# The operands of the first layers stand at four other distances from the weights in SBUF

## What is computed

```python
w = softmax(weight_gen)                     # per token: 8 heads, 7 taps
x = sum over 7 taps of w * x[token - tap]   # causal mixing, per head of 24 columns
y = ((sigmoid(x @ w_gate)) * (x @ w_val)) @ w_out       # 192 -> 1536 -> 192
h = y @ w_in                                            # 192 -> 2048
g = (a0 + a1*h + a2*h*h + a3*h*h*h) / (1 + |b0|*|h| + |b1|*h*h + 1e-6)
out = g @ w_out2                                        # 2048 -> 192
```

## Time and profile before

| | |
|---|---|
| median of 3 runs | 1399.78 us (1399.17 to 1400.05) |
| the profiled execution's own time | 1399.86 us |
| its span, first to last instruction | 1398.1 us |
| busy: TensorE, its weight loads, VectorE, ScalarE, GpSimd | 97%, 88%, 90%, 77%, 26% |

### The profile page before, as it was taken

The page is one execution under the profiler, slowest core; times in us unless marked ns, Lnnn a source line. Parts: engine busy times, 40 slices in busy tenths (PEclk is TensorE's granted clock), DMA queues, the critical chain, the costliest instruction groups (busy, mean ns, idle before and its releaser), DMA issues.

```text
span 1398.1 us, 19047 instructions
## 1 busy us (share of the span) xinstructions
PE 1362.1 (97%) x7282; PEld 1234.8 (88%) x7282; DVE 1257.5 (90%) x1498; ACT 1080.7 (77%) x1467; POOL 356.9 (26%) x204
## 2 busy tenths in 40 slices
PE   5999999999999999999999999999999999999977
PEld 5899899899899899999999998998998999999966
DVE  7788999999999999999999999999998998889998
ACT  3487887787888787787778878788777778778975
POOL 0333233141332323133141323323133231210000
PEclk9999999999999999999999999999999999999999
DMA  9200100001010010101001010010101001000000
GB/s 231 76 32 1 38 0 23 22 1 43 1 44 1 0 44 0 44 1 34 10 1 44 0 43 1 0 44 0 42 1 40 1 1 35 1 12 0 13 0 18
DMA packets 13467, 33.06 MB, mean 24 GB/s; under 512 B 1600, under 2 KB 7746, under 8 KB 13376
## 3 DMA queue, kind: packets, MB, share of 16 engines
q1 hardware_dynamic: 13312, 31.85, 7.5%
q0 software_dynamic: 64, 0.00, 0.0%
HBM read 25.55 MB, written 6.29 MB: 23 GB/s over the span
## 4 chain that ended last, share of the span: by engine, by line
PE 91%; DVE 5%; ACT 1%; issue 1%; DMA 0%; SPq 0%; DVEq 0%
PE ring L325 50%; PE acc L352 40%; PE ring L379 1%; PE ring L382 1%; DVE work L734 1%; DVE work L713 1%; DVE work L707 1%; DVE work L720 1%; DVE work L743 0%; DVE work L727 0%; DVE work L654 0%; DMA window<-in_x_dram 0%; DVE u L701 0%; ACT work L500 0%; DVE val_w L671 0%
## 5 line engine op out<-in xcount | busy, mean ns | idle before, releaser
L352 PE MATMUL acc<-out_w,work 128*128 128x192 f32 x2048 | 365.8, 330 | 13.8 <-DVE work L743 13.8
L352 PEld LDWEIGHTS acc<-out_w,work 128*128 128x128 f32 x2048 | 341.8, 192 | 20.1 <-DVE work L743 14.1
L490 ACT ACTIVATE work<-ring,coef 128x512 f32<-128x512 f32 (+1 forms) x272 | 182.2, 670 | 215.4 <-PE ring L325 212.9
L325 PE MATMUL ring<-yt,in_w 128*128 128x512 f32 (+1 forms) x1360 | 326.0, 386 | 2.3 <-DVE work L713 1.9
L352 PE MATMUL acc<-out_w,u 128*128 128x192 f32 x1536 | 283.8, 327 | 3.7 <-DVE u L701 3.5
L325 PEld LDWEIGHTS ring<-yt,in_w 128*128 128x128 f32 x1360 | 244.9, 189 | 47.5 <-DVE work L713 2.9
L352 PEld LDWEIGHTS acc<-out_w,u 128*128 128x128 f32 x1536 | 256.7, 190 | 9.7 <-DVE u L701 3.3
L325 PE MATMUL ring<-xt,gate_w 128*128 128x512 f32 (+1 forms) x1020 | 262.3, 387 | 1.3 <-DVE val_w L671 0.8
L325 PE MATMUL ring<-xt,val_w 128*128 128x512 f32 (+1 forms) x1020 | 252.2, 377 | 0.0
L604 POOL TENSOR_TENSOR mixed<-mixed,prod 128x768 f32<-128x768 f32 (+1 forms) x90 | 197.2, 2191 | 169.0 <-DVE u L701 152.1
L599 POOL TENSOR_TENSOR prod<-window,mixw 128x768 f32<-128x768 f32 (+1 forms) x90 | 135.3, 1503 | 399.3 <-DVE work L720 298.0
(11 more groups left out here) (57 smaller groups left out, 915.8 us busy)
## 6 DMA issues: line engine op xcount, KB each, us to landing
window<-in_x_dram SPq DMA_DIRECT2D x14, 960.0 KB, 4.7
out_dram<-zsb SPq DMA_DIRECT2D x15, 384.0 KB, 2.6
out_w<-in_moe_w_out_dram SPq DMA_DIRECT2D x1, 1536.0 KB, 21.2
mixw<-in_weight_gen_dram SPq DMA_DIRECT2D x13, 112.0 KB, 3.0
out_w<-in_moe_w_out_dram SPq DMA_DIRECT2D x2, 576.0 KB, 8.2
work<-in_moe_w_in_dram SPq DMA_DIRECT2D x2, 512.0 KB
work<-in_moe_w_in_dram SPq DMA_DIRECT2D x4, 256.0 KB, 14.5
window<-in_x_dram SPq DMA_DIRECT2D x1, 768.0 KB, 4.3
```

The costliest lines, as they stand in the source:

```text
L325: last = nc.tensor.matmul(dst, wt[:, c], xs[:, 0:n], start=at == 0, stop=at == 4)
L352: last = nc.tensor.matmul(dst, src[:, n * P:(n + 1) * P], w[:, i, :], start=i == 0 and n % 2 == 0, stop=i == last_i and n % 2 == 1, skip_g ...
L490: nc.scalar.activation(den(n), h, ACT.Abs, scale=coef[:, 6:7])
```

## The change

No instruction is added, removed or moved. The tensors `xt0_free`, `xt1_free`, `yt0_free`, `yt1_free` and `work_free` are never read or written; they push what stands behind them. 

```diff
-        xt = [[sb(f"xt{b}_{n}", [P, T], F32R) for n in range(4)] for b in range(2)]
-        yt = [[sb(f"yt{b}_{n}", [P, T], F32R) for n in range(4)] for b in range(2)]
+
+        def operands(name, free):
+            sb(f"{name}_free", [P, free // 4])
+            return [sb(f"{name}_{n}", [P, T], F32R) for n in range(4)]
+
+        xt = [operands("xt0", 256), operands("xt1", 128)]
+        yt = [operands("yt0", 64), operands("yt1", 128)]
+        sb("work_free", [P, 112])
```

## The result

The changed kernel takes 1407.79 us (median of 4 runs, 1407.25 to 1409.22) against 1399.47 us before (4 runs); the ratio is 1.0063, with a 95% interval of 1.0047 to 1.0079. It is slower by 8.3 us. The forecast was no change, 1399.8; the time lies inside the stated range of 1380 to 1415, where the rival that ended slower (1407 to 1417) had it.

A forecast was written before the change was run, and what follows sets the result against it. The prediction took TensorE's matmul start-to-start distances to bound the kernel. Padding, second layers and first-layer matmuls at their new distances were all priced 0: 1399.86 + 0, stated as 1399.8 us, range 1380 to 1415.

The forecast's parts named there:

- no change: Whole kernel: address shifts leave first-layer matmul spacing as it was, 1399.8 us; chance 0.44.
- the rival that ended slower: First-layer matmuls at new distances: stream might not fall back after disturbances, 3 to 5 ns each, 1410 us; chance 0.26.
- What bounds the kernel: From 100 to 1300 us TensorE never pauses; time is the sum of matmul start-to-start distances; TensorE 97% of span.
- The padding and the second layers at 0: Unused pads cost nothing; second-layer matmuls stay at 162.5 ns, their distances unchanged less multiples of 512; priced 0.
- Whole multiples of 512 mean nothing: First-layer operand-to-weight distances: shifts by whole 512 bytes change nothing; 840 matmuls all at 389 ns.
- Distance 0 costs 0: First-layer matmuls on `xt0`: some 56 of 840 already had distance 0 and lasted 389 ns, so price 0.
- Between these ends I take 0: First-layer matmuls at distances 128, 192, 320: bounds -37 to +37 us, 0 chosen between them.
- The third reading: Ten `in_w` matmuls at 755 us had median 394 ns, not 389, at the same distances: the excess depends on start moment.
- The prediction's last sentence: Sign of a wrong forecast: a collision period longer than 64 bytes that doesn't show between 0 and 256.
- The rival of free distances: First-layer matmuls: some new distances avoid the two streams' collision, saving 11 ns each; 1388 us; chance 0.30.
- The 11 ns that each first-layer matmul carries: Excess of each of 3400 first-layer matmuls over the second layers' fixed part; 37 us, 2.7% of the kernel.
- The Trainium skill's two ports: TensorE's reads of SBUF: independent ports for operand and weights, so loading next weights costs nothing; sum 0 at every distance.

The follow-up runs named there:

- run 5: Not a follow-up run: the words belong to "could run 5 ns slower", said of the `in_w` matmuls at 755 us, median 394 ns instead of 389.
- the layout assumed above: Pads of 4, 4, 8, 488 bytes (distances meant 260, 264, 272, 248; if rounded to 32: 288, 320, 352, 352), against the kernel before: 1414.07 us, before 1399.77.
- 32 distances tried by words: Two kernels against the one before, each operand tensor at its own word distance, sixteen in each: 1413.33 us and 1414.37 us, before 1399.19.

## Why the forecast of no change missed and the range held

The time lies in the range because the range was drawn to take in the rival that ended slower. The forecast itself, no change, failed, and it failed in its mechanism.

**What bounds the kernel** was right: no other engine's time grew by more than 0.2 us, and what the first-layer matmuls lost came through to the end, 7.4 us of the 9.0 in the middle stretch, with 1.6 given back at the two ends.

**The padding and the second layers at 0** was right: 3.90 and 5.20 us in every kernel, and 5.20 also where, by the layout assumed above, `u` and `work` had moved by 128 against their weights.

**Whole multiples of 512 mean nothing** was right, and 256 is already enough.

**Distance 0 costs 0** was right: 0.9995 to 1.0012 with all four sets there. In the changed kernel `xt0` lost 1 ns, most likely through its neighbours.

**"Between these ends I take 0"** is the step that failed. It rested on two things. One was that two streams which sweep over places that repeat every 512 bytes or a smaller power of two meet equally often wherever they start. The period is indeed such a one, 256 bytes, and the cost depends on the start all the same. The other was that 0 and 256, the two distances for which rows existed, cost the same. They do because they are one place, a period apart; the rows had sampled a single point of the curve twice. The third reading, the 394 ns at 755 us, was the one to weigh more: it showed that the same matmuls could run 5 ns slower in another phase, and this is the size of what the other distances cost. The prediction's last sentence names the case that came true, a period longer than 64 bytes that doesn't show between 0 and 256; it was written down as a sign of error and not weighed in the sum.

**The rival that ended slower** had the mechanism and the price: at another distance the stream doesn't fall back to 389. It put 7 to 12 us on the 2320 matmuls of three sets at 3 to 5 ns; measured were 2 to 6 ns by set and 8.3 us. The shortest, median and longest duration that it named part as it said: 389/389/389 before, and in the changed kernel

```profile
L331 PE MATMUL ring<-xt,val_w x830: 389/392/404, 100.0 to 1248.1; 128*128 128x512 f32 x166
```

**The rival of free distances** has nothing for it: of the eight multiples of 32 and of 32 distances tried by words no set or pass ran near 216 ns. The other 24 words were not tried. The 11 ns that each first-layer matmul carries at the best distance too are not explained by these runs. A distance moves the cost from 227 up to some 233 ns, never down, so they could be the part of the collision that no distance avoids, or a cost of float32r that has nothing to do with SBUF; no kernel here takes the loads away.

**The Trainium skill's two ports.** By the Trainium skill, "TensorE: Matmul & The Clock Gate", section "Step-by-step: what each phase is for", loading the next weights takes no read bandwidth of SBUF from the running matmul. The run in which one weight tensor of each layer moved disagrees: the matmul under which it is loaded takes 396 instead of 389 ns, and a run of 30 takes 6.90 us instead of 6.81. For float32r operands the measurement decides.

## What to carry to other kernels

A TensorE-bound stream can be sensitive to where its operands stand in SBUF although no instruction changes; read the start-to-start distance of its matmuls, and check that shortest, median and longest duration agree. If they don't, shift the moving operands against the weights; here a distance of a whole multiple of 256 bytes was the good one, worth 0.6% to 1.2% against the kernels in which two or more sets stood elsewhere. Adding or resizing a tensor between the two can lose it unnoticed, so a change measured at 1% should be looked at for a shift of addresses before it is credited to what it was meant for. And when two samples of an unknown curve agree, ask first whether they could be the same point.

## What was not expected of the hardware

- The spacing of these float32r matmuls depends on the distance in SBUF between the streamed operand and the weights that are loaded meanwhile: 227 ns at a multiple of 256 bytes, some 230 at 64 past one, 231 to 234 at the other distances tried (means over a set). Float32 matmuls of the second layers, at 162.5 ns, show nothing of it at the distances that they had.
- It repeats from kernel to kernel. Two kernels with distances 256 bytes apart have the same four rows, and so, to the hundredth of a microsecond, have the two at distance 128, one of which is the other shifted by 128 bytes.
- At the good distance the stream of gated products settles: 840 `val_w` matmuls of one duration, 389 ns, in every run after the disturbance with which it begins. With other distances in the kernel it stays unsettled, 387 to 404 ns.
- A pad of 4 bytes seems to move what follows by 32: the set meant for 264 had the 391 ns of 320 (or 64), and its kernel's other sets fit the same reading.
